# Sliding-window attention feeding two feed-forward stages: transposes issued ahead of the value matmuls, and an output's low part taken ahead of the masks

## The reference

```python
scores = scale * np.matmul(q, k.transpose(0, 1, 3, 2))
keep = is_sink | in_window            # pos < 4, or 0 <= rel < 128
scores = np.where(keep, scores, -1000000000.0)
scores = scores - np.max(scores, axis=-1, keepdims=True)
a = np.exp(scores)
a = a / (np.sum(a, axis=-1, keepdims=True) + 1e-09)
x = np.matmul(a, v)                   # (tokens, 512) after a reshape
...
g = h * np.tanh(softplus(h)), h = x @ w_in;  x = g @ w_out
...
out += p[:, e:e + 1] * (np.maximum(x @ w1[e], 0.0) @ w2[e])   # 4 experts
```

## Time and profile before

| | us |
|---|---|
| median of 3 runs | 852.86 (852.78 to 852.87) |
| span of the profiled execution | 851.0 |
| TensorE busy in it | 842.8 (99%) |
| VectorE, ScalarE, GpSimd busy | 605.4, 401.6, 172.1 |
| attention's steady part, from 11.84 to 81.18 | 69.34: TensorE busy 69.34, ScalarE 63.59, VectorE 59.59, GpSimd 53.93 |

### The profile page before, as it was taken

One profiled execution on the slowest core, in us unless ns is written; L12 is line 12 of the kernel. 1 busy time (PEld: TensorE's weight loads), 2 busy tenths in 40 slices (PEclk: granted clock), 3 DMA queues, 4 the chain that ended last, 5 costly groups with the idle time before them and its releaser, 6 DMA issues.

```text
span 851.0 us, 13888 instructions
## 1 busy us (share of the span) xinstructions
PE 842.8 (99%) x4518; PEld 729.6 (86%) x4518; DVE 605.4 (71%) x1170; ACT 401.6 (47%) x739; POOL 172.1 (20%) x259
## 2 busy tenths in 40 slices
PE   7999999999999999999999999999999999999998
PEld 5777888888888888898999899889989998999897
DVE  7888799898888989876566565565565555656655
ACT  6999754448754549754324314314414413422410
POOL 6778200001100112222012112102202202202100
PEclk9999999999999999999999999999999999999999
DMA  7555730004830006825045135225225315403304
GB/s 257 143 162 154 159 100 1 1 0 97 194 106 0 0 0 127 162 59 115 19 104 117 28 89 117 43 74 117 56 61 117 68 49 117 92 25 68 69 0 151
DMA packets 25622, 72.70 MB, mean 85 GB/s; under 512 B 4336, under 2 KB 6512, under 8 KB 25584
## 3 DMA queue, kind: packets, MB, share of 16 engines
q0 software_dynamic: 10720, 33.82, 22.1%
q1 hardware_dynamic: 14576, 38.04, 13.1%
q10 hardware_dynamic: 288, 0.39, 0.1%
HBM read 35.28 MB, written 3.15 MB: 45 GB/s over the span
## 4 chain that ended last, share of the span: by engine, by line
PE 99%; DMA 0%; POOL 0%; DVE 0%; ACT 0%; issue 0%; SPq 0%; DVEq 0%
PE banks L944 31%; PE banks L870 28%; PE banks L839 15%; PE banks L636 15%; PE banks L651 3%; PE banks L732 3%; PE banks L702 3%; PE banks L738 1%; DMA pool<-kT 0%; POOL pool L480 0%; PE banks L705 0%; PE banks L957 0%; ACT pool L1067 0%; DVE pool L1863 0%; DVE pool L1486 0%
## 5 line engine op out<-in xcount | busy, mean ns | idle before, releaser
L1789 DVE SCALAR_TENSOR_TENSOR pool<-banks,p_norm,pool 128x512 f32<-128x512 f32 x179 | 132.8, 748 | 66.1 <-PE banks L944 64.3
L944 PE MATMUL banks<-w_hi,g_lo 128*128 128x512 f32 x382 | 149.9, 392 | 0.0
L944 PE MATMUL banks<-w_lo,g_hi 128*128 128x512 f32 x382 | 149.7, 392 | 0.0
L944 PE MATMUL banks<-w_hi,g_hi 128*128 128x512 f32 x382 | 148.7, 389 | 0.0
L1291 ACT ACTIVATE g_hi<-pool 128x384 fp32r<-128x384 f32 x96 | 50.5, 526 | 190.7 <-DVE pool L1769 139.1
L870 PE MATMUL banks<-x_hi,w_lo 128*128 128x384 f32 x256 | 86.0, 336 | 0.0
L870 PE MATMUL banks<-x_hi,w_hi 128*128 128x384 f32 x256 | 85.9, 335 | 0.0
L870 PE MATMUL banks<-x_lo,w_hi 128*128 128x384 f32 x256 | 85.7, 335 | 0.0
L944 PEld LDWEIGHTS banks<-w_hi,g_lo 128*128 128x128 f32 x382 | 71.7, 188 | 15.0
L944 PEld LDWEIGHTS banks<-w_hi,g_hi 128*128 128x128 f32 x382 | 71.7, 188 | 13.8 <-issue 0.2
L944 PEld LDWEIGHTS banks<-w_lo,g_hi 128*128 128x128 f32 x382 | 71.7, 188 | 13.8
(11 more groups left out here) (151 smaller groups left out, 1776.3 us busy)
## 6 DMA issues: line engine op xcount, KB each, us to landing
w_raw<-weights SPq DMA_DIRECT2D x48, 512.0 KB, 4.4
w_lo<-w_raw POOLq DMA_DIRECT2D x48, 512.0 KB, 5.5
w_lo<-w_sum POOLq DMA_DIRECT2D x15, 384.0 KB, 4.0
pool<-v SPq DMA_DIRECT2D x8, 384.0 KB, 3.5
out<-pool SPq DMA_DIRECT2D x11, 256.0 KB, 2.0
pool<-kT SPq DMA_DIRECT2D x7, 400.0 KB, 5.0
pool<-qT SPq DMA_DIRECT2D x7, 384.0 KB, 4.1
w_lo<-pool POOLq DMA_DIRECT2D x2, 384.0 KB, 4.9
```

The costliest lines, as they stand in the source:

```text
L944: mm = pe.matmul(banks[:, bank, :], g[:, s, f * SUP + at:f * SUP + at + P], w_cols(w, p2 * SLOT + DOWN_AT[f], DM), start=(f == 0 and n == ...
L1789: dve.scalar_tensor_tensor(out=to, in0=d_bank, scalar=share, in1=to, op0=ALU.mult, op1=ALU.add)\
```

## The change

```diff
@@ TensorE, window_attention, period(ct, g, before)
                     scores(ct, g)
+                    if at := group_at(ct, g, TURN_LAG, before):
+                        turn(*at)
                     if at := group_at(ct, g, VALUES_LAG, before):
                         values(*at)
-                    if at := group_at(ct, g, TURN_LAG, before):
-                        turn(*at)
@@ VectorE, window_attention, period(ct, g, before)
                     if copied:
                         copy_second(*copied)
+                    if ended and not first_half:
+                        take_after(*ended)
                     mask_scores(ct, 4 * g)
                     mask_scores(ct, 4 * g + 1)
-                    if ended and not first_half:
-                        take_after(*ended)
                     if at := group_at(ct, g, 1, before):
                         invert(at[0], 4 * at[1], 4)
```

## The result

| | us |
|---|---|
| before, measured beside it | 852.87 (852.78 to 852.87, 4 runs) |
| after | **857.15** (857.07 to 857.22, 4 runs) |
| after / before | 1.0051, interval 1.0038 to 1.0065 |
| span of the profiled execution | 855.3 (before 851.0) |

The changed kernel is 4.3 us slower, and it was forecast at 857.1. The page's part 1 of after answers to the earlier trace rows: TensorE has the same 4518 instructions.

What follows compares the result with a forecast made beforehand. TensorE, busy 99% of the span, was taken as the bound, so waits act one to one. Terms 0.2 + 3.4 + 0.6 = 4.2 on 851.0 gave 855.2, with 1.9 around it 857.1 us; range 854.8 to 858.4.

Steps and rivals of the forecast that it cites:

- end of attention: TensorE's last period closes with values instead of turn, losing the cheap step from transposes to dense matmuls: +0.17 us.
- six turns of B: Turn in periods B of groups 7 to 22 waits for GpSimd: 0.51 plus 0.06 each, +3.4 us.
- start: Turn in period 3 waits for GpSimd's multiplications at its fifth transpose: 0.58 + 0.06, +0.6 us.
- change-overs, 21 periods: TensorE's three changes of matmul kind per period with both turn and values: sum taken as unchanged.
- Part 1: Order on TensorE: three change-overs a period, sum unchanged; +0.17 us where attention ends.
- rivals 3 and 4: Turn to values free: 3 gives 854.1 us, chance 0.09; 4, with GpSimd also in time, 850.7, chance 0.05.
- the free step: 128x128 transposes go to the sinks' 128x64 transpose at no price; applied to turn-to-values it would save 3.0 us.
- Part 2: Turn due earlier waits for GpSimd: 0 in A and C, 0.23 or 0.38 us late in B.
- Part 3: VectorE's moved subtraction waits for ScalarE in A, making invert 0.28 late and B's turns wait: +3.4 us.
- rival 2: Tight places of period A, with 0.1 to 0.2 slack, give way too: 858.3 us, chance 0.08.
- Part 4: Start: turn in period 3 waits for GpSimd, +0.6 us; that lateness then covers the first B.
- Rival 1: The subtraction isn't waited for, only GpSimd's own lateness counts in B: 855.9 us, chance 0.18.

Runs made afterwards that it cites:

- turn alone: The change with turn ahead of values on TensorE, but VectorE's subtraction back in its old place behind the first two masks: 855.63 us, ratio 1.0034.
- the last experiment: The kernel before, with turn(22) directly behind the first dense step and values(21) behind the second, ahead of values(22): 852.49 us, ratio 0.9997.
- the start mended: The change, but with values ahead of turn in period 3 alone, as before: 856.76 us, ratio 1.0047.

## Why the prediction was right

The parts of the loss, by the starts of phases in the trace of after:

| | predicted | measured |
|---|---|---|
| end of attention | 0.17 | 0.20 |
| six turns of B | 3.4 (0.57 each) | 3.0 (0.51 and 0.49) |
| every second batch, turn of A and scores of B | 0 | 0.6 |
| start | 0.6 | 0.63 |
| change-overs, 21 periods | 0 | 0 |
| sum | 4.2 | 4.4, in the span 4.3 |

**The bound.** TensorE had no wait to absorb anything, so each wait went one to one to the end. The kernels' times fit the sums of their phases within 0.15 us (turn alone: 2.9 against 2.8; B in its old order: 0.63 + 0.20 + 0.24 + 0.34 = 1.41 against 1.43).

**Part 1.** Right: the sum of three change-overs is unchanged, in C 0.80 and 1.46 for turn and values as before. Values start 0.20 behind the last transpose and not 0.11, so rivals 3 and 4 fall. The row that I set against the free step, dense matmuls to values, was the one to go by. The free step from 128x128 to 128x64 transposes didn't carry over to values. Between transposes and dense matmuls a change-over is free as well, as the last experiment shows.

**Part 2.** GpSimd is late in B, as worked out, and in time in C. But the part's own sizes, 0.23 and 0.38 with the subtraction in its old place, were not confirmed: there turn of B is only 0.08 longer. What failed is "GpSimd keeps its distance to the scores". With the old order on VectorE, turn of A is itself 0.18 to 0.34 late, which delays the scores of B, and so GpSimd is 0.86 ahead of them and not 0.68 (in the other kind of batch 0.86 and not 0.53). The 0.23 less 0.18 leaves 0.05, and the 0.38 less 0.33 (0.86 - 0.53) leaves 0.05; with the restart it is 0.08. The waits in A and in B are two prices for one lateness of VectorE, and I added them as if each stood alone. The sentence that the old place of the subtraction is "0.1 late" in A was under-sized too: it is 0.18 to 0.34. The subtraction ends at the same distance to the scores of A as before (55.17 - 53.44 = 1.73, before 53.43 - 51.68 = 1.75), but what waits for it is the load of the eighth transpose's weights, which stands 0.1 ahead of the transpose and starts 0.05 behind the subtraction's end (55.23); and in the other kind of batch the subtraction is 0.15 later.

**Part 3.** Right in each step, and 0.06 to 0.08 too much in its total. ScalarE's `x_hi` sets the subtraction in five of the six A (predicted to start 0.11 behind its end, measured 55.25 - 55.10 = 0.15), GpSimd starts 0.43 ahead of the scores of B (predicted 0.4), and the fifth transpose comes 2.06 behind them (predicted 56.57 - 54.48 = 2.09). Turn of B is 0.51 or 0.49 longer with the restart in it, where I had 0.51 and 0.06 more. Moving the subtraction costs more in B than it saves in A, as said: 1.5 us in all. The experiment that undoes B's order (3.0 us back) and the one that puts a mask and `invert` earlier (3.2 back) both confirm that these waits are the loss.

**What was missed.** I took the batches to be alike. In those whose A is a first period of the loop, VectorE is later against TensorE: its second mask starts 0.40 behind the first instead of 0.28 (66.03 to 66.43; 55.59 to 55.88), the third starts 0.24 ahead of the scores of B (67.23 against 67.47) instead of 0.40, and the scores, which reuse the masked banks, take 0.08 to 0.13 more. I had named who waits behind the moved instruction as masks, `invert` and GpSimd, but not TensorE's scores, which wait for the masks. It is 0.34 in all. Three turns of A take 0.08 more, 0.24 in all: that much of rival 2 came true, a fifth of its size. Why VectorE is later there isn't shown. What holds the three turns is the way from GpSimd's copy of the sinks to the load of the eighth transpose's weights. GpSimd, the last register instruction in TensorE's queue and the load, in the batch at 65 us:

```profile
65.84 0.24 POOL L495 COPY pool<-pool 128x64 f32<-128x64 f32 x1
...
L701 PEldq ALU_OP  x1: 32/32/32, 66.2 to 66.2; - x1
...
66.29 0.14 PEld L702 LDWEIGHTS banks<-ident,pool 128*128 128x128 f32 x1
```

The copy ends at 66.08. Two register instructions (L698 at 66.11, L701 at 66.21) run between it and the load, which starts 0.21 behind the copy's end. In the batch at 55 us only one runs there, and the load starts 0.12 behind. In the change, in the kernel with B in its old order and in the one with a mask ahead of the subtraction, the three late turns of each all have 0.21 or 0.22 there, while the distance to the end of the subtraction runs from 0.18 to 0.27; so it is the copy and not `x_lo`. That is what rival 2 named as its condition. The 0.4 for B that is too much and this 0.6 make the total agree better than its terms do.

**Part 4.** Right: 0.63, and the first B is covered by it. With the start mended, 0.26 came back in period 4.

**The rivals.** Rival 1 asked whether the subtraction is waited for; VectorE's waits for `x_hi`, in five of the six A, say yes. Rival 2 came true in three of six A. Rivals 3 and 4 fall with the 0.20 of values.

## What to carry to other kernels

Where the bounding engine never waits, moving one of its steps ahead buys nothing, as long as no change-over gets cheaper by it, and spends the slack of everyone who feeds it: lay each feeder's end against a fixed phase, and check the steps that reuse its buffers as well as those that read its results. An instruction with a wait of its own, put at the head of an in-order queue, delays all that stands behind it, and it belongs behind work that is ready: here one mask ahead of the subtraction, with `invert` directly behind it, was enough. Two lateness terms that feed the same engine one after the other don't add: the first gives the second its time (turn of B 0.08 longer, where 0.29 and 0.44 were added).

## What the runs showed of the hardware

- A VectorE instruction of four columns (`TENSOR_SCALAR`) took 0.47 to 0.59 instead of 0.16 in five periods in which it began while GpSimd was multiplying, ending 0.02 to 0.03 behind GpSimd's end. I had not expected the size of the instruction to be no protection.
- The price of changing the kind of matmul depends on the pair. From transposes to values it is 0.09 between the starts (0.20 for 0.11), from dense matmuls to transposes nothing (0.23 for 0.23), and from values to dense matmuls 0.10: the last four value matmuls take 0.32 to the dense one in the trace of after (85.27 to 85.59), where four take 0.22 to further values (60.23 to 60.45).
- A semaphore can reach TensorE through more than one register instruction, and each adds 0.09: the load behind them started 0.21 behind GpSimd's end with two, 0.12 with one.
